# A table of places for the first instructions of every engine in a fused top-k attention and two-block MLP kernel

## The reference

```python
scores = q @ k.T / sqrt(64)                    # 4 batches x 8 heads, 576 tokens each
kth    = the 32nd largest score of each row
scores = where(scores >= kth, scores, -1e9)    # keep the top 32 of each row
attn   = softmax(scores)
x      = attn @ v                              # regrouped to 2304 tokens x 512

h = x @ w_in;  g = h * sigmoid(h);  x = g @ w_out          # 512 -> 2048 -> 512
a = x @ w1;  b = x @ w2;  out = ((a * b) @ w3) @ w_out2    # 512 -> 1024 -> 512
```

## Time and profile before

| | us |
|---|---|
| median of 3 runs | 1113.53 (1113.38 to 1116.69) |
| the profiled execution | 1112.51 |
| its span | 1110.7 |
| PE busy | 1048.4 |
| DVE busy | 931.9 |
| ACT busy | 775.7 |
| POOL busy | 619.6 |

### The profile page before, as it was taken

One profiled execution on the slowest core, in us unless ns is written; L12 is line 12 of the kernel. 1 busy time (PEld: TensorE's weight loads), 2 busy tenths in 40 slices (PEclk: granted clock), 3 DMA queues, 4 the chain that ended last, 5 costly groups with the idle time before them and its releaser, 6 DMA issues.

```text
span 1110.7 us, 24334 instructions
## 1 busy us (share of the span) xinstructions
PE 1048.4 (94%) x7872; PEld 982.2 (88%) x7872; DVE 931.9 (84%) x2066; ACT 775.7 (70%) x1921; POOL 619.6 (56%) x803
## 2 busy tenths in 40 slices
PE   2998698999999999999999999999999999999998
PEld 1554598999999999999999999999999999999897
DVE  4999998989999999999998999999999999981110
ACT  3888888768776777787767776877677767774221
POOL 3777889666654555566544556665455445543211
PEclk9999599999999999999999999999999999999999
DMA  8998999969995898699858996999579748954962
GB/s 247 338 319 292 320 305 370 317 203 327 362 333 175 284 336 298 206 335 363 312 174 288 336 301 201 314 352 350 179 269 341 253 150 308 319 204 149 340 213 95
DMA packets 129053, 310.42 MB, mean 279 GB/s; under 512 B 14240, under 2 KB 43936, under 8 KB 128928
## 3 DMA queue, kind: packets, MB, share of 16 engines
q1 hardware_dynamic: 128928, 308.86, 80.6%
HBM read 263.19 MB, written 45.61 MB: 278 GB/s over the span
## 4 chain that ended last, share of the span: by engine, by line
PE 71%; DMA 11%; DVE 10%; issue 2%; ACT 2%; SPq 2%; POOL 1%; ACTq 0%; POOLq 0%; DVEq 0%
DMA win<-win_split 9%; PE ps_h L1033 6%; PE ps_h L1035 6%; PE ps_h L1034 6%; PE ps_s L929 5%; PE ps_x L965 5%; PE ps_h L995 5%; PE ps_y L1017 5%; PE ps_y L1019 5%; PE ps_y L1018 5%; PE ps_h L996 5%; PE ps_h L997 4%; DVE top L828 4%; PE ps_t L944 4%; PE ps_y L1046 3%; DVE rest L830 3%
## 5 line engine op out<-in xcount | busy, mean ns | idle before, releaser
L828 DVE MAX8 top<-rest 128x8 f32<-128x576 f32 x432 | 312.9, 747 | 0.0
L668 POOL TENSOR_TENSOR g_lo<-gate,g_hi 128x256 fp32r<-128x256 f32 x216 | 159.6, 739 | 181.8 <-ACT g_hi L796 180.3
L830 DVE MATCH_REPLACE8 rest<-top,rest 128x576 f32<-128x576 f32 x288 | 212.5, 743 | 0.5
L995 PE MATMUL ps_h<-x_hi,win 128*128 128x256 f32 x576 | 166.9, 290 | 12.7 <-DMA win<-win_split 12.7
L1033 PE MATMUL ps_h<-x_hi,w_hi 128*128 128x256 f32 x576 | 165.5, 287 | 4.5 <-DVE x_lo L884 4.5
L656 POOL TENSOR_TENSOR pT<-p_raw,pT 128x640 fp32r<-128x640 f32 x72 | 113.3, 1573 | 100.6 <-ACT pT L756 100.2
L1017 PE MATMUL ps_y<-g_hi,wout 128*128 128x256 f32 x576 | 164.9, 286 | 0.6 <-POOL g_lo L668 0.6
L1035 PE MATMUL ps_h<-x_hi,w_lo 128*128 128x256 f32 x576 | 162.7, 282 | 0.0
L1034 PE MATMUL ps_h<-x_lo,w_hi 128*128 128x256 f32 x576 | 162.7, 282 | 0.0
L996 PE MATMUL ps_h<-x_lo,win 128*128 128x256 f32 x576 | 162.1, 281 | 0.0
L997 PE MATMUL ps_h<-x_hi,win 128*128 128x256 f32 x576 | 162.0, 281 | 0.0
(11 more groups left out here) (78 smaller groups left out, 2780.9 us busy)
## 6 DMA issues: line engine op xcount, KB each, us to landing
win<-win_split SPq DMA_DIRECT2D x135, 512.0 KB, 6.5
wout<-wout_split SPq DMA_DIRECT2D x135, 512.0 KB, 5.0
wout<-w_dram SPq DMA_DIRECT2D x72, 512.0 KB, 3.8
v_split<-v_dram SPq DMA_DIRECT2D x64, 320.0 KB, 5.6
k_split<-k_dram SPq DMA_DIRECT2D x64, 288.0 KB, 5.9
v_dram<-v_split SPq DMA_DIRECT2D x32, 320.0 KB, 6.0
k_raw<-kT SPq DMA_DIRECT2D x64, 144.0 KB, 5.1
k_dram<-k_split SPq DMA_DIRECT2D x32, 288.0 KB, 4.5
```

The costliest lines, as they stand in the source:

```text
L668: nc.gpsimd.tensor_tensor(g_lo[:, n % NR, :], gate[:, n % NG, :], g_hi[:, n % NR, :].bitcast(F32), ALU.subtract).then_inc(g_split, 1)
L828: nc.vector.max(best[:, 8 * n:8 * n + 8], sc if step == 0 else left).then_inc(topk_step, 1)
L830: nc.vector.match_replace(left, best[:, 8 * n:8 * n + 8], sc if step == 1 else left, BELOW_ALL).then_inc(topk_step, 1)
L995: nc.tensor.matmul(ps_h[:, f % 2, 0:UN], hi, xh, start=(c == 0), stop=False)
```

## The change

The order functions no longer only sort. They hand their list to `in_order`, which looks each operation up in `FIRST_PLACES`, a table of place numbers by engine and kind (the n-th entry is the place of the n-th operation of that kind). Operations that have a place come first, in the order of their places; the rest follow, sorted by position as before. The table covers all that an engine does up to about the middle of the second unit's H and Y blocks: 213 places on PE, 422 on DVE, 374 on ACT, 222 on POOL, 249 on SP. `TOP_SPAN` and nearly all lags have new values as well, and these set the order behind the table. No operation is added or removed, no semaphore wait is changed.

```diff
-TOP_SPAN = 0.902
+TOP_SPAN = 0.875
 
 LAG = {
-    "Q": -3.056, "K": -3.841, "KB": -2.505, "V": -1.013, "VB": -0.536, "KS": -0.987, "VS": 2.763, "WS": 1.1,
...
+    "Q": -3.157, "K": -3.785, "KB": -2.751, "V": -1.016, "VB": -0.473, "KS": -1.067, "VS": 2.763,
...
+FIRST_PLACES = {
+    "tensor": {
+        "QK": (0, 1, 2, 3, 4, 8, 14, 18, 24, 28, 34, 38, 44, 48, 54, 58, 64, 66, 68, 71, 73, 76, 78, 87,
...
+    "scalar": {
+        "KR": (0, 5, 6, 19, 23, 37, 53, 69, 219, 254, 279, 296, 311, 332, 355, 373,),
...
+def in_order(engine, out):
+
+    first, rest, seen = [], [], {}
+    for at, op in sorted(out, key=lambda o: o[1][1:]):
+        places = FIRST_PLACES.get(engine, {}).get(op[0], ())
+        n = seen[op[0]] = seen.get(op[0], -1) + 1
+        if n < len(places) and places[n] >= 0:
+            first.append((places[n], op))
+        else:
+            rest.append((at, op))
+    return sorted(first, key=lambda o: o[0]) + sorted(rest, key=lambda o: o[0])
 
 def pe_order():
...
-    return sorted(out, key=lambda o: o[0])
+    return in_order("tensor", out)
```

More of the change, by code:

```diff
@@ L169 @@
 MLP_AT = mlp_positions()
-TOP_SPAN = 0.902
+TOP_SPAN = 0.875
 LAG = {
-    "Q": -3.056, "K": -3.841, "KB": -2.505, "V": -1.013, "VB": -0.536, "KS": -0.987, "VS": 2.763, "WS": 1.1,
-    "WS_PACE": 0.863, "WS_LATE": 0.215, "LOD": 1.852, "WS_KEPT": -0.204, "W12": 7.488, "W12_PACE": 0.773,
[8 rows of a table removed]
-}
+    "Q": -3.157, "K": -3.785, "KB": -2.751, "V": -1.016, "VB": -0.473, "KS": -1.067, "VS": 2.763,
+    "WS": 1.062, "WS_PACE": 0.863, "WS_LATE": -0.216, "LOD": 1.852, "WS_KEPT": -0.228, "W12": 7.491,
[8 rows of a table added]
+}
+FIRST_PLACES = {
+    "tensor": {
[15 rows of a table added]
+    },
+    "vector": {
+        "DEN": (23, 41, 60, 79, 98, 118, 137, 156, 174, 196, 220, 241, 261, 279, 299, 320, 331, 363,
+            386, 407,),
+        "RDEN": (24, 42, 61, 80, 99, 119, 138, 157, 175, 197, 221, 242, 262, 280, 300, 321, 332, 364,
+            387, 408,),
+        "LO": (35, 54, 73, 92, 111, 130, 148, 167, 186, 207, 229, 250, 271, 301, 324, 338, 356, 375,
+            395, 416,),
+        "W34": (38, 53, 69, 87, 102, 115, 131, 146,),
+        "XS": (48, 67, 86, 105, 124, 143, 162, 181, 201, 224, 247, 267, 293, 316, 333, 351, 373, 389,
+            410,),
+        "G": (189, 193, 198, 203, 209, 217, 225, 231, 238, 245, 246, 264, 265, 274, 278, 285, 358, 366,
+            370, 376, 379, 384, 393, 397, 403, 412, 417,),
+        "X2": (297, 298,),
+        "BM": (304, 310, 318, 327, 330, 339, 345, 353,),
+        "TOP": (0, 1, 2, 3, 4, 5, 6, 7, 8, 9, 10, 11, 12, 13, 14, 15, 16, 17, 18, 19, 20, 21, 22, 25,
[15 rows of a table added]
+    },
+    "scalar": {
+        "KR": (0, 5, 6, 19, 23, 37, 53, 69, 219, 254, 279, 296, 311, 332, 355, 373,),
+        "QR": (1, 2, 7, 21, 31, 46, 63, 79, 89, 104, 120, 135, 144, 172, 191, 218, 251, 264, 277, 297,
+            316, 347, 365,),
+        "SC": (3, 4, 11, 13, 20, 24, 34, 40, 48, 56, 68, 72, 83, 87, 98, 103, 113, 117, 130, 131, 142,
+            143, 162, 169, 185, 190, 208, 216, 232, 235, 249, 252, 260, 265, 287, 295, 304, 310, 324,
+            331, 343, 351, 362, 369,),
+        "MASK": (15, 16, 25, 28, 41, 43, 58, 59, 73, 74, 92, 93, 107, 109, 125, 126, 137, 138, 148, 151,
+            177, 178, 201, 202, 220, 223, 240, 242, 255, 256, 270, 271, 286, 288, 306, 308, 330, 338,
+            353, 357, 371,),
+        "VR": (8, 22, 35, 51, 64, 81, 96, 106, 282, 292, 318, 329,),
+        "EXP": (17, 18, 29, 30, 44, 45, 61, 62, 76, 78, 94, 95, 110, 111, 127, 128, 139, 140, 154, 160,
[19 rows of a table added]
+    },
+    "gpsimd": {
+        "KR": (0, 3, 4, 11, 18, 25, 37, 46, 149, 160, 171, 181, 189, 200, 215,),
+        "QR": (1, 2, 5, 12, 19, 28, 39, 48, 57, 65, 76, 86, 92, 117, 132, 137, 157, 162, 168, 182, 191,
+            206, 217,),
+        "BOUNDS": (9, 17, 26, 33, 45, 56, 64, 74, 84, 91, 107, 122, 135, 148, 159, 165, 174, 187, 199,
+            210, 220,),
+        "VR": (6, 15, 24, 34, 44, 53, 62, 75, 177, 185, 197, 214,),
+        "NORM": (13, 14, 22, 23, 30, 31, 42, 43, 51, 52, 60, 61, 69, 70, 81, 82, 88, 89, 100, 104, 114,
[10 rows of a table added]
+    },
+    "sync": {
[6 rows of a table added]
+        "RAW": (0, 2, 1, 3, 21, 29, 31, 37, 40, 47, 51, 55, 59, 61, 68, 71, 78, 83, 88, 91, 95, 102,
+            106, 111, 124, 134, 130, 143, 140, 151, 148, 159,),
+        "WSK": (22, 30, 32, 38, 41, 48, 52, 56, 60, 62, 69, 72, 79, 84, 89, 93, 96, 103, 107, 112, 125,
[7 rows of a table added]
+        "WIN": (120, -1, 126, -1, 133, -1, 142, -1, 155, -1, 162, -1, 167, 177, 178, 179, 214, 218, 220,
+            225, 228, 230, 232, 236, 240, 245, 248,),
+        "WOUT": (129, -1, 136, -1, 145, -1, 154, -1, 161, -1, 169, -1, 174, 180, 183, 184, 191, 195,
+            198, 202, 205, 208, 213, 215, 223, 226, 227, 229, 231, 235, 238, 244, 247,),
+    },
+}
@@ L241, in act_order @@
             out += [(p + LAG["OC"], ("OC", u, 0)), (p + LAG["OC"] + 0.01, ("OC", u, 1))]
-    return sorted(out, key=lambda o: o[0])
+    return in_order("scalar", out)
 def pool_order():
@@ L257, in pool_order @@
             out.append((p + LAG["GLB"], ("GL", FC12 * u + FC1 + f)))
-    return sorted(out, key=lambda o: o[0])
+    return in_order("gpsimd", out)
 def dve_order():
@@ L277, in dve_order @@
             out += [(p + LAG["X2L"], ("X2", u, 0)), (p + LAG["X2L"] + 0.01, ("X2", u, 1))]
-    return sorted(out, key=lambda o: o[0])
+    return in_order("vector", out)
 def sp_order():
@@ L312, in sp_order @@
                 out += [(p + LAG["OUT"], ("OUT", u, 0)), (p + LAG["OUT"] + 0.01, ("OUT", u, 1))]
-    return sorted(out, key=lambda o: o[0])
+    return in_order("sync", out)
 def build(nc, qT, kT, vx, w_in, w_out, w1, w2, w3T, wo2, out):
```

## The result

The changed kernel takes 1117.53 us (median of 20 runs, 1114.14 to 1121.25); the old one took 1113.93 beside it (20 runs, 1110.12 to 1119.67). The ratio is 1.0033, with a 95% interval of 1.0019 to 1.0047: slower by 3.6 us, where 3.2 us of gain were forecast, and outside the range given.

The account below looks back on a forecast made before the run. The end was taken as PE finishing unit 0, with DVE full in the opening, plus 8 units at PE's pace. 1112.51 - 2.7 - 0.5 = 1109.3 us, as a median 1110.3; range 1104.5 to 1115.5.

Parts of the forecast that it names:

- 3, SC5: Opening, ACT: K4's split ahead of score copy SC5 makes DVE wait, giving back 2.7 of 4.8 us.
- Step 2: Opening, DVE: TOP instructions placed ahead of LO0 hide its wait, 0.7 us gained; its 1.0 us of work only moves.
- step 1: Opening, ACT: first score copies ahead of the second keys' rounding, so DVE starts 4.8 us sooner.
- Step 4: First H block of unit 0: sooner by 2.5 to 3 us, mainly through the POOL hand-over to XL3.
- Step 5: First H to first A block, unit 0: DVE's X2 ends last; A block 1.1 us sooner.
- rival D: Unit 0: PE waits longer for DVE and its clock falls, costing 4 us, sum 1114.4; chance 0.04.
- Step 6: QK 32 and 33 done before the first A block save 1.6 us; unit 1 starts 2.7 us sooner.
- Step 7: Unit 1 to the end: PE's waits for win loads may shift; gain 0.5 us, bounds 3 either side.
- C: Unit 0 and start of unit 1: weight loads come late on SP, 8 us lost, 1118.3; chance 0.11.
- B: Unit 0: DVE's lead is lost again to waits that push X2; no change, 1113; chance 0.25.

Follow-up runs that it names:

- e6: Old kernel without DEN, the addition of EPS to the row sums: 1108.65 us, ratio 0.9954 to the old kernel.
- e5: Changed kernel without DEN, the addition of EPS to the row sums: 1103.39 us, ratio 0.9911 to the old kernel.
- e8: Old kernel with ACT's first two score copies moved ahead of the split of K1: 1112.76 us, ratio 1.0003 to the old kernel.
- e9: Changed kernel with DEN written as a sum over the pair of row sum and EPS: 1106.96 us, ratio 0.9946 to the old kernel.
- e10: Changed kernel with the old lags behind the table and without DEN: 1105.03 us, ratio 0.9928 to the old kernel.
- e1: Changed kernel with the old lags and TOP_SPAN behind the table: 1115.2 us, ratio 1.0037 to the old kernel.
- e7: Changed kernel with the splits of K4 and K5 moved back on ACT: 1117.67 us, ratio 1.0049 to the old kernel.
- e12: Old kernel without DEN, with two early score copies on ACT and five DVE operations moved later: 1119.9 us, ratio 1.0071 to the old kernel.

## Why the prediction was wrong

The seven steps, held against the pair without DEN (e6 as before, e5 as after), which takes DEN out on both sides:

| step | foretold | measured without DEN | measured with DEN |
|---|---|---|---|
| 1, first max | 4.8 sooner, at 9.4 | 5.3 sooner, 9.27 | 4.9 sooner, 9.30 |
| 3, SC5 | copied by 33.8, a wait for K4 | starts 33.40, wait 3.13 | starts 33.20, wait 3.08 |
| 4, first H | 2.8 sooner | 2.1 sooner | 2.1 later |
| 5, first A | 1.1 sooner | 1.2 sooner | 6.2 later |
| 6, first H of unit 1 | 2.7 sooner | 2.6 sooner | 4.8 later |
| 7, end (span) | 3.2 sooner | 2.9 sooner | 6.3 later |

*Steps 1 to 3.* Right: the second lane of step 2 was put at 33.8 and started at 33.86. The load of K5 was overlooked, a term of 2.05 us on DVE that the sum does not have. Step 2 was priced as a wait of 0.7 us; e8 shows it to be a condition of step 1, which leaves the sum as it is.

*Step 4 failed*, at the sentence "the number of instructions does not change, so the lead stays 2.8", and with it the one ahead of all steps, "as only the order is changed, every duration stays". The number did stay. The durations did not: up to the first H block DEN takes 5.80 us instead of 2.05, and these 3.75 us are most of the 4.2 between the two columns above. Its second half, the hand-over on POOL, was right: from XS7 to the first H block it is 2.2 us in e5 against 5.4 in e6, 3.2 us gained where 2.3 were foretold. XS7 itself comes 1.15 us later in e5 than in e6 (130.01 against 128.86), not 0.5 sooner. So that the pair comes near the forecast of 2.8 is in part luck: the missing K5 and the hand-over lie on opposite sides.

*Step 5* failed too, and DEN is the smaller part of it. DVE's work from the second lane of step 2 to X2 was put at 169.9 us and 1 of waits, and took 178.2 (33.86 to 212.02). In it DEN is 2.9 us longer than before (7.28 against 4.43), and the waits are not 1 us but 6.9: 2.05 for the x copy in the opening, then 2.5 for scores and 2.3 for the gate in unit 0. In e5 this stretch takes 168.5 us with 5.3 of waits, in e6 166.1 with 10.7. This tells why DEN costs so much more in the changed kernel. In the old one DVE waits for others anyway, 8.2 us, and when DEN's 4.4 go 2.4 of them come back as waits. The changed order has 12 TOP instructions more there and fewer waits to hide in; when its 7.3 us go, the waits do not grow, and X2 comes 9.5 us sooner. The forecast of 1.1 us for the first A block agrees with the pair's 1.2 by luck as well, since both sides of that pair have other waits than the forecast had.

From first H to first A the changed kernel needs 74.7 us, e5 71.2, e9 72.6, the old kernel 70.6. Of the 3.5 us between the changed kernel and e5 DEN's own length is 1.6 (in the old kernel it is 2.5 in this stretch, so DEN alone does not make it longer than the old one's), and a fall of the clock an estimated 1.3 (rival D below). The rest was not separated; one candidate is the clock behind the first H block, 0.86 up to 150 us in the changed kernel and 1.00 in e5.

*Step 6* was right: from first A to the first H block of unit 1 it is 42.7 us against 44.1, in the pair without DEN as well.

*Step 7.* The waits for win fell by 4.7 us, those for DVE grew by 4.3, and 1.4 for wout came. From the first H block of unit 1 to the end the changed kernel takes 861.5 us, the old one 860.0, and without DEN they take 856.3 and 856.6. All in all, taking DEN out is worth 9.5 us at the first A block and 14.6 in the span of the changed kernel (1117.0 against 1102.4), and 2.0 and 5.4 in the old one (1110.7 against 1105.3). The difference of 9.2 turns the 2.9 us of gain into the 6.3 of loss that the profiled executions show; by the medians the loss is 3.6.

*The rivals.* C did not happen; in unit 0 no wait for win shows at all. B, a lead lost in unit 0, has the right place in part, and DVE's waits there are part of the cause. D happened in a small way: PE waited 1.32 and 0.53 us at 191.12 and 192.41, and the granted clock of 190 to 200 us is 0.83, where e5 keeps 1.00:

```profile
190.00:200.00 10.00, 9.20 (x77) 9.03 (x76) 9.83 (x23) 8.13 (x22) 9.57 (x12) 1.00 1.04 301
```

It is not tied to DEN. e9 and e10, which have no long DEN, show the same fall (0.57 in both from 184 to 188 us), and e1 and e7, in which DEN is long, keep 1.00 from 150 to 211 us. What it costs can be read from e10 and e5, which have the same lists up to there and differ in this fall: from first H to first A 72.5 us against 71.2, so some 1.3 us, an estimate from two executions. Nor do these traces tell when the clock falls: from 182 to 184 us PE is busy 0.83 of 2 us in e5 and 0.85 in e9, with waits of 1.02 and 0.52 us in the one and 1.17 and 0.54 in the other, and only in e9 does the clock fall behind it.

What I could have seen beforehand: the views of the old kernel's DEN give a mean of 271 ns and a longest of 1166, where the shortest is 147. An instruction on 128x2 elements with such a spread is being held by something, and the new order was free to make it worse. The Trainium skill has the rule, in "SBUF — State Buffer", "Who interferes with whom": GpSimd and some kinds of DVE instruction share one pair of ports, held for a whole instruction, so that the second to start stands until the first is through; a `tensor_scalar` can be of these kinds, a `tensor_reduce` on this chip never is. The traces agree on both: in the changed kernel 31 long DENs, each ending with the POOL instruction, and in e9 72 short ones as a sum. That the ports are the reason stands on the page; the runs show which kind of instruction is held and until when.

## What to carry to other kernels

A change of order leaves the work the same but not its length: list every instruction whose longest duration is far above its shortest, see which other engine's instruction it ends with, and ask where the new order puts the two. What such an instruction costs depends on the waits around it: in the old order part of it fell into waits for others, in the new one nearly none. On the path that sets the end it may be better written as another kind, or left out, than scheduled around; here that beats both kernels, at 1103.39 us without the addition and 1106.96 with it as a sum. And a wait that goes is worth its length only if what stands behind it in each list is ready; a single early head (e8), or one engine's moves without the others' (e12), brought nothing or harm.

## What the runs showed of the hardware

- The granted clock of PE fell within unit 0 to 0.83 over 10 us (190 to 200 us of the changed kernel), behind two waits of 1.32 and 0.53 us; PE was busy 0.76 of the 2 us from 190 to 192. A like dip in e5 had no fall behind it.
